# A mixer-and-MLP kernel on one core: weight pieces of the first chunk staged up to four steps later, and one weight product moved ahead of the gates' transpose

## What is computed

```python
# _attn_ref, per batch and head, for every step t
m_new = np.maximum(f_gate + m, i_gate)
C = exp(f_gate + m - m_new) * C + exp(i_gate - m_new) * outer(v, k)
n = exp(f_gate + m - m_new) * n + exp(i_gate - m_new) * k
y = sigmoid(o_gate) * (C @ q) / maximum(abs(n @ q), 1.0)
# _moe_ref, then _moe2_ref, on the [3072, 320] result
x = ((x @ w1) * (x @ w2)) @ w3 @ w_out
out = maximum(maximum(x @ m1, x @ m2), x @ m3) @ m_out
```

## Time and profile before

| | |
|---|---|
| median of 3 launches | 690.27 us (689.67 to 695.02) |
| the profiled launch | 692.49 us |
| its span on the core | 690.8 us |
| PE busy | 680.7 us (99%), 3456 matmuls |
| PEld busy | 565.3 us (82%) |
| DVE busy | 395.3 us (57%) |
| ACT busy | 284.6 us (41%) |
| POOL busy | 119.4 us (17%) |
| mean DMA rate | 95 GB/s over the span, 65.70 MB |

### The profile page before, as it was taken

How to read it: one execution, slowest core, us unless ns; L and a number is a source line. 1 busy time by engine, 2 the same in 40 slices (tenths; PEclk the granted TensorE clock), 3 DMA queues, 4 the chain that set the end, 5 groups by cost and what they waited for, 6 DMA issues and landing times.

```text
span 690.8 us, 10625 instructions
## 1 busy us (share of the span) xinstructions
PE 680.7 (99%) x3456; PEld 565.3 (82%) x3456; DVE 395.3 (57%) x855; ACT 284.6 (41%) x600; POOL 119.4 (17%) x155
## 2 busy tenths in 40 slices
PE   8989999999999999999999999999999999999997
PEld 5877888888888888888888888888888888887785
DVE  7558889754667733676743576753567743322422
ACT  1456756333645412664422555422545422322211
POOL 3423243020134200043300044200023100000000
PEclk9999999999999999999999999999999999999999
DMA  7988687060544410455410245510155100100001
GB/s 218 315 267 214 145 218 182 27 156 1 143 125 126 114 39 0 103 141 138 121 37 0 86 127 136 142 40 0 47 149 122 45 1 1 38 1 0 1 1 38
DMA packets 39077, 65.70 MB, mean 95 GB/s; under 512 B 4180, under 2 KB 21908, under 8 KB 39044
## 3 DMA queue, kind: packets, MB, share of 16 engines
q1 hardware_dynamic: 38676, 64.83, 34.5%
q10 hardware_dynamic: 368, 0.44, 0.2%
HBM read 58.00 MB, written 4.03 MB: 90 GB/s over the span
## 4 chain that ended last, share of the span: by engine, by line
PE 94%; DVE 2%; DMA 2%; ACT 1%; SPq 0%; issue 0%; DVEq 0%; ACTq 0%
PE ring L515 54%; PE acc L515 24%; PE ybank L515 10%; PE sbank L515 3%; DMA qk_s<-in_qkT 1%; PE tbank L515 1%; PE tbank L606 1%; DVE gm L1037 1%; DVE hid L1056 1%; ACT gm L745 0%; DMA g_i<-in_ig 0%; DVE x1T L1156 0%; SPq L314 0%; ACT c_part L745 0%; ACT left L745 0%
## 5 line engine op out<-in xcount | busy, mean ns | idle before, releaser
L515 PE MATMUL ring<-x1T,mx_hi 128*128 128x512 f32 x432 | 152.9, 394 | 0.3 <-ACT left L745 0.2
L515 PE MATMUL ring<-xT,ab_hi 128*128 128x512 f32 x384 | 136.6, 396 | 0.0
L745 ACT ACTIVATE gm<-hid 128x512 fp32r<-128x512 f32 x84 | 53.1, 632 | 166.3 <-DVE hid L1056 129.7
L477 POOL TENSOR_TENSOR decay_s<-decay_s,causal 128x512 f32<-128x512 f32 x41 | 53.8, 1311 | 383.3 <-DMA qk_s<-in_qkT 368.8
L515 PE MATMUL acc<-gm,wp 128*128 128x512 f32 x384 | 97.1, 395 | 0.4 <-DVE gm L1037 0.4
L515 PEld LDWEIGHTS ring<-x1T,mx_hi 128*128 128x128 f32 x432 | 81.1, 188 | 18.4 <-ACT left L745 0.7
L745 ACT ACTIVATE left<-ring 128x512 f32<-128x512 f32 x84 | 49.9, 594 | 92.0 <-PE ring L515 92.0
L515 PEld LDWEIGHTS acc<-gm,wp 128*128 128x128 f32 x384 | 71.6, 188 | 16.7 <-ACT gm L745 0.8
L1037 DVE TENSOR_TENSOR gm<-hid,gm 128x512 fp32r<-128x512 f32 x84 | 58.2, 692 | 46.0 <-ACT gm L745 46.0
L515 PE MATMUL ring<-x1T,mx_lo 128*128 128x512 f32 x216 | 84.2, 390 | 0.0
L515 PEld LDWEIGHTS ring<-xT,ab_hi 128*128 128x128 f32 x384 | 72.2, 188 | 14.5 <-ACT xT L745 0.2
(11 more groups left out here) (150 smaller groups left out, 920.4 us busy)
## 6 DMA issues: line engine op xcount, KB each, us to landing
qk_s<-in_qkT SPq DMA_DIRECT2D x40, 480.0 KB
decay_s<-phi_d SPq DMA_DIRECT2D x41, 256.0 KB, 4.4
kg_s<-in_kg SPq DMA_DIRECT2D x40, 160.0 KB, 5.5
vn_s<-in_vn SPq DMA_DIRECT2D x48, 84.0 KB, 2.1
w_raw<-in_w3T SPq DMA_DIRECT2D x7, 512.0 KB, 6.7
out_y<-stage SPq DMA_DIRECT2D x12, 256.0 KB, 2.2
c_st<-c_part SPq DMA_DIRECT2D x24, 105.0 KB
stage<-in_wmax SPq DMA_DIRECT2D x6, 384.0 KB, 3.9
```

Of the source, the lines that this page charges most:

```text
L477: pool.tensor_tensor(d4, d4, causal[:].unsqueeze(1).broadcast_to([P, HQ, L]), ALU.add).then_inc(s["masked"], 1)
L515: return pe.matmul(o, l, r, start=start, stop=stop)
L745: return act.activation(o, i, ACT.Copy)
```

## The change

It moves work between places of the same programs; no instruction is added or taken away. SP: the six ab pieces are issued at k = 3 (piece 0), k = 4 (1 and 2), k = 6 (3) and k = 7 (4 and 5) instead of k = 2 (0 and 1) to k = 6 (5), and piece 6 moves from k = 7 to the front of pieces 7 and 8 in `body(0)`. ACT: `piece_hi` 0 at k = 4, 1 and 2 at k = 5, 3 at k = 6, 4 at k = 7 and 5 after the loop. DVE: `piece_lo` 0 at k = 5, 1 and 2 at k = 6, 3 and 4 at k = 7, and 5 after the last `gate_out`. TensorE: `product_step(0, 0)` moves ahead of `turn_gates`.

```diff
+        early_loads = [[], [], [], [0], [1, 2], [], [3], [4, 5]]
+        early_hi = [[], [], [], [], [0], [1, 2], [3], [4]]
+        early_lo = [[], [], [], [], [], [0], [1, 2], [3, 4]]
...
                 if k == 2:
-                    load_piece(0)
                     sp.wait_ge(s["rest_ok"], 4 + REST)
...
-                load_piece(k - 1)
+                for n in early_loads[k]:
+                    load_piece(n)
...
                     if isinstance(c, int) and c == 0 and k == 1:
-                        for n in range(QUADS - 1, N_AB + NSTAGE):
+                        for n in range(N_AB, N_AB + NSTAGE):
                             load_piece(n)
...
             mm(acc[1][:], ident[:], causal[:].unsqueeze(1).broadcast_to([P, HQ, L]), True, False)
+            product_step(0, 0)
             pe.wait_ge(s["stack_ok"], 3)
...
             last.then_inc(s["decay_ok"], 1)
-            product_step(0, 0)
...
-                if k >= 2:
-                    piece_hi(k - 2)
+                for n in early_hi[k]:
+                    piece_hi(n)
             first_out(QUADS - 1)
+            piece_hi(N_AB - 1)
             x_hi(0, 0)
...
                     weigh(0, k)
-                    if k >= 3:
-                        piece_lo(k - 3)
+                    for n in early_lo[k]:
+                        piece_lo(n)
                     normaliser(0, k - 1)
                     gate_out(0, k - 1)
-            piece_lo(N_AB - 1)
             normaliser(0, QUADS - 1)
             gate_out(0, QUADS - 1)
+            piece_lo(N_AB - 1)
             x_lo(0, 0)
```

## The result

The changed kernel takes **696.21 us** as the median of 20 launches (691.7 to 702.03), and the kernel before, launched beside it, 689.73 us (20 launches, 688.9 to 695.19): a ratio of 1.0091, with a 95% interval of 1.0072 to 1.011. The change makes the kernel 6.5 us slower. I had forecast 686.8 us, 3.5 us faster, so the sign was wrong.

The account below looks back on a forecast made before the run. PE, busy 680.7 of 690.8 us, was taken as the bound, so only its gaps and slow stretches count. 1.82 + 1.89 + 0.36 - 0.6 = 3.5 us off the 690.27 us median gave 686.8 us, range 685.8 to 690.2.

Parts of the forecast that it names:

- Quad 4's wait, 1.82: At quad 4's scores: with two 512 KB pieces no longer ahead of `qk_s`, PE's whole wait of 1.82 us goes.
- its clock, 1.89: Behind quad 4's wait: the slow PE clock over scores and product passes goes with the wait, gaining 1.89 us.
- rival A: Start of the program: plain launches wait too little to lower the clock; gain only 1.6 us, 688.7 us; chance 0.2.
- The product step, 0.36: Before the gates' transpose: the moved product step fills PE's wait for DVE, gaining 0.36 us, bounds 0 and 0.36.
- Nothing, but with only 0.4 us or a little more in hand: Quad 5's keys: landing by 40.4 us, wanted at 40.8, so no cost; other bound a 1 us wait.
- rival B: The wait moves to quad 5's scores: gain 2.5 us, or 0.6 if the clock falls, 687.8 to 689.7; chance 0.15.
- Piece 4's landing and the loop's end, 0.6: End of first loop: late pieces delay DVE's chain into block 1; PE loses 0.6 us, bounds 0.1 and 4.0.
- L: Piece 4's time to landing at the loop's end: taken as 4.0 us; PE loses max(0, L - 3.4).
- rival C: Loop's end: late pieces are on the path; with L of 7.4 us, 1.8 us slower, 692.1 us; chance 0.08.
- Pieces 6 to 8 in `body(0)`: Start of block 1: later piece 6 and 128 KB more ahead of chunk 1's quad 0 cost nothing.
- All that depends on PE shifts with it: End of first loop: old-trace times may be used, since everything that depends on PE moves along with it.
- a gap under 1 us cost only itself: PE clock after short waits: gaps under 1 us bring no slow clock; 1.9 us kept for the range.

Follow-up runs that it names:

- a1: Kernel before with only the first product step moved ahead of the gates' transpose: 690.49 us, ratio 1.0007.
- a2: The full change without the move of the product step, so the pieces alone: 701.26 us, ratio 1.0157.
- c4: Kernel before with only pieces 3 to 8 as late as in the change; pieces 0 to 2 and product step in their old places: 689.77 us, 0.999.
- d1: c4 with piece 2 issued at k = 4 instead of k = 3: 692.09 us, ratio 1.0027.
- d3: c4 with pieces 1 and 2 both issued at k = 4, piece 0 at k = 2: 697.8 us, ratio 1.0113.
- b3: b1 with piece 2 moved from k = 4 to k = 5, behind quad 5's loads: 693.28 us, ratio 1.0049.
- b1: The full change with pieces 6 to 8 loaded at quad 3 of chunk 1 instead of quad 1, splits two steps later: 696.34 us, ratio 1.0091.
- b0: The full change itself measured again, beside b1, b2 and b3: 701.21 us, ratio 1.0159.
- b2: Kernel before with two extra, unread 512 KB transfers at the end of SP's first loop: 695.0 us, ratio 1.006.
- d2: The full change with piece 2 issued at k = 5, pieces 6 to 8 still in front of `c_st`: 698.43 us, ratio 1.009.
- a4: Kernel before with only piece 6 moved from quad 7 to `body(0)`: 689.27 us, ratio 0.9986.
- a3: The full change with pieces 6 to 8 loaded behind the `c_st` transfers, splits of pieces 6 to 12 a step later: 696.61 us, ratio 1.0094.
- c3: b2 with one extra 512 KB transfer instead of two: 690.34 us, ratio 0.9998.
- c1: Kernel before with pieces 0 to 2 as in the change, 3 to 6 at k = 5 to 7, product step unmoved: 699.62 us, ratio 1.0155.
- c2: As c1, but pieces 0 to 6 issued at k = 3, 4, 5, 5, 6, 7, 7: 692.28 us, ratio 1.0022.

## Why the prediction was wrong

**The cause, as far as it is shown.** The loss is in the pieces (a1, a2), and it does not come without the first half of their move: 0 KB of pieces 0 to 2 moved gives 0.999 (c4), 512 KB 1.0027 (d1), 1,024 KB 1.0113 (d3). Two waits make up most of it in the traces. One is at quad 5, shown by taking it away (b3 against b1, 3.1 us). The other is for `c_st`: moving 1,152 KB out from in front of it gives 4.9 us (b1 against b0, whose own trace lacks the wait), it can be made by 1,024 KB more in front of it (b2), and it stands without a wait at quad 5 (d2). A third, shorter one is at `xT` at the start of block 1: none in after, 0.7 us in d1, 1.0 in b0, 1.2 in d3. What joins the first half of the move to the late landing of `c_st` is not shown. Missing DMA time fits the trace of after and doesn't fit those of d1 and d2, and no run changed the holes alone.

**Point by point.**

1. *Quad 4's wait, 1.82, and its clock, 1.89.* In the trace both are gone, as forecast: the scores start at 33.94 with no wait. **The term was right for the profiled launch and wrong for the median**, to which I applied it. The lowest launch of before is 688.9 us, a1's profiled launch waits 0.84 us with no slow clock, a4's not at all. 692.49 - 3.71 is 688.8, which is where the lowest launches of before lie, and 12 of its 20 lie under 690: most of them will not have had the 3.7 us. This is rival A, and it was underrated at 0.2: the 2.2 us between the profiled launch and the median are most simply read as this wait.

2. *The product step, 0.36.* Right in this trace, nothing measurable in the median (a1). Its lower bound was too kind: in the profiled launches of a3, d2 and b3 PE waits 0.56, 0.68 and 1.12 us at the moved step for the piece of `w_out`, more than the 0.36 us that it won. In the old order the transpose and the row selection stand ahead of the step, and a2, which keeps it, has no wait for that piece in its trace.

3. *"Nothing, but with only 0.4 us or a little more in hand" at quad 5.* Wrong, and rival B right: 0.91 us in the profiled launch of after, 1.3 in b0's, 1.6 in d3's, 1.9 in b1's and a2's, the last two with the clock down. I had counted the bytes ahead (512 KB less than before) and not that they now come in one lump of 1,024 KB within 1.7 us directly ahead of the queries: `qk_s` took 8.35 us to land. With 512 KB ahead there was no wait (b3, d1, d2).

4. *Piece 4's landing and the loop's end, 0.6.* In after L was 3.73 us against my 4.0, and the loss 0.28 us, near the L - 3.4 of the sum. In b0's profiled launch L was 4.56 and PE lost 1.4 us there, so the term is larger in some launches. This is where rival C put its price, with 7.4 us; that was not the mechanism. The Trainium skill's rule that stood beside C (DMA: Bandwidth & Descriptors, "Rules for kernel authors": issue early, wait late) pointed to the right side all the same, though no transfer of the late half was lost by its fixed cost, and c4, which has four of them late, loses nothing.

5. *"Pieces 6 to 8 in `body(0)` ... Cost nothing; the cover is several microseconds on both."* **This is the step that failed most.** I looked at who uses the moved pieces and at quad 0 of chunk 1, and not at what is queued behind them on SP: `c_st`, which PE needs at 72.4. I also misread the queue: "128 KB more ahead of it (512 for 384)" counts one piece, but pieces 4 and 5 both stand there now, 1,024 KB where piece 6 had 384. Moving piece 6 costs nothing alone (a4), and neither does the whole late half (c4); but `c_st` had only about 1.4 us to spare (c3), and with the first half moved too it lands later than that. The term is 2.45 us of wait and 1.89 of clock in the profiled launch; 3.4 to 7.5 us of wait in b2, a2, d1 and d2.

6. *"All that depends on PE shifts with it".* I reckoned in the times of the old trace. In after PE wants the state 2.97 us earlier than before, and the state lands later, at 74.79, where in before the DMA engines are idle from 73 us on (share 0.01). So the landing did not shift with PE. PE's gain alone is not the reason: a1, a4 and c4 reach the state at 71.85, 71.34 and 72.35 us, as early as after, and don't wait.

The lower end of my range has a slip besides: 690.27 - 4.07 - 0.6 is 685.6, not 685.8.

**What stays open.** What makes `c_st` land late once the first half is moved. How long each of the waits is in a plain launch: only one launch of each kernel has a trace, and in b0 and d3 it was the lowest, without the wait for `c_st`. The mean granted clock, which is on record for every launch, says a little: over the 20 launches of after it falls from 1.000 in the lowest (691.7 us) to 0.989 in the highest (702.03), with a median of 0.996, against 0.999 in the launches of before beside the experiments. So the slower launches of after hold slow stretches too, and its lowest, at full clock, is still 2.0 us over the median of before. Why the rate falls at a full share: from 62 to 66 us c4 moves 295 GB/s at a share of 1.07, d2 189 at 1.05. And how much of c1 is the first half and how much SP's held queue.

No kernel tried here beats the one before by more than the measurement can tell; a4 and c4, at 0.9986 and 0.999, come nearest.

## What to carry to other kernels

Before moving transfers later, list everything that is behind them in the same queue up to the next quiet stretch of the DMA, with the time at which each is wanted; the one that is hurt need not be near the edit. Leaving DMA engines idle early may be a cost if they are full later. That is a thing to check and not a result of these runs: the bytes counted over the windows fit one of three traces. And take the size of a wait from more than one launch before subtracting it from a median: if the profiled launch lies over the median, the wait may be just that difference.

## What the runs showed of the hardware

**A full DMA has no one rate.** At a share of 1.0 to 1.07 these traces show from 189 GB/s (d2, 62 to 66 us) to some 350 (353 in the earlier trace rows), so a busy share does not say how many bytes go through. The 160 KB of queries took from 4.98 us (c1) to 10.57 us (c2) to land. The Trainium skill's line for one transfer (DMA: Bandwidth & Descriptors, "Anatomy of one DMA", fitted on the GpSimd path) gives an estimate of 3.2 us for 512 KB; piece 4 took 3.73 in after, with the engines half busy (share 0.48 from 49 to 54 us), and 4.56 in b0's profiled launch.

**The PE clock after short waits.** The granted clock stayed at 1.00 behind waits of 0.84 (a1), 0.91 (after), 1.07 (c1), 1.3 (b0), 1.59 (d3) and 2.11 us (b3, at 124.33). It fell behind 0.71 (b1, at 100.19), 1.21 (a3), 1.29 (c2), 1.82 (before) and 1.9 us (b1, a2). Behind the waits for `c_st` of 2.45 us and more it always fell, which cost 1.9 us in after; after 3.4 us in b2 `attend` alone took 3.41 instead of 1.59. So up to 2 us the length of the wait does not tell whether the clock falls. The prediction let a gap under 1 us cost only itself; behind the 0.71 us in b1 the clock averages 0.66 over 5 us, an estimated 1.7 us lost, more than twice the wait. The launches of after spread by 10 us.
